# A routed two-layer mixture of experts: the second routing test of a phase written out among an expert's products, and the close of a phase split over two experts

## The reference, cut to what matters

```python
def _moe_ref(x, w_gate, w1, w2):          # N 3072, D 320, E 8, F 1024
    cap = N // E                          # 384
    flat = (x @ w_gate).flatten()
    for idx in np.argsort(-flat):         # greedy over all (token, expert) pairs
        tok, e = idx // E, idx % E
        if assigned[tok] >= 0 or counts[e] >= cap: continue
        assigned[tok] = e; counts[e] += 1
    for e in range(E):
        mask = assigned == e
        out[mask] = np.maximum(x[mask] @ w1[e], 0) @ w2[e]
```

## Time and profile before

| | |
|---|---|
| median of 3 runs | 870.5 us |
| lowest and highest | 869.16, 877.2 us |
| the profiled execution | 880.63 us |
| its span | 878.9 us |
| PE busy | 729.0 us (83%) |
| DVE, ACT, POOL busy | 529.1, 290.1, 413.2 us |
| mean granted TensorE clock | 0.90 of full speed |

### The profile page before, as it was taken

One profiled execution on the slowest core, in us unless ns is written; L12 is line 12 of the kernel. 1 busy time (PEld: TensorE's weight loads), 2 busy tenths in 40 slices (PEclk: granted clock), 3 DMA queues, 4 the chain that ended last, 5 costly groups with the idle time before them and its releaser, 6 DMA issues. The chain is left out here.

```text
span 878.9 us, 17001 instructions
## 1 busy us (share of the span) xinstructions
PE 729.0 (83%) x5044; PEld 672.5 (77%) x5044; DVE 529.1 (60%) x1622; ACT 290.1 (33%) x756; POOL 413.2 (47%) x557
## 2 busy tenths in 40 slices
PE   0999999994328795986959799983899998999897
PEld 0899999993217684866847698982899997999896
DVE  6479999985775556555556545445546364464462
ACT  4222222220014241422314246451524254245241
POOL 6568878871043452352426375874224043242341
PEclk9999999996558897897779799996899998999999
DMA  8857666625431411223221424535462424623610
GB/s 272 190 148 191 193 186 187 179 79 171 115 130 29 145 48 45 91 87 95 87 73 50 132 66 140 180 105 161 158 206 73 145 70 116 201 81 124 186 33 17
DMA packets 99641, 109.59 MB, mean 125 GB/s; under 512 B 39053, under 2 KB 83726, under 8 KB 99568
## 3 DMA queue, kind: packets, MB, share of 16 engines
q1 hardware_dynamic: 85792, 74.83, 29.8%
q10 hardware_dynamic: 9696, 21.24, 7.5%
q0 software_dynamic: 4080, 12.61, 4.5%
HBM read 89.45 MB, written 20.02 MB: 125 GB/s over the span
## 5 line engine op out<-in xcount | busy, mean ns | idle before, releaser
L535 POOL TENSOR_TENSOR parts_w2l<-all_w,parts_w2h 128x320 fp32r<-128x320 f32 x128 | 113.5, 903 | 131.2 <-ACT parts_w2h L522 128.2
L595 DVE SCALAR_TENSOR_TENSOR l_hl<-bank,l_hh 128x384 fp32r<-128x384 f32 (+1 forms) x168 | 83.1, 494 | 137.6 <-ACT l_hh L591 134.9
L591 ACT ACTIVATE l_hh<-bank 128x384 fp32r<-128x384 f32 (+1 forms) x168 | 74.0, 440 | 167.5 <-PE bank L576 163.0
L572 PE MATMUL bank<-l_xh,parts_w1h 128*128 128x384 f32 x256 | 94.8, 370 | 23.1 <-DVE l_xh L565 12.6
L573 PE MATMUL bank<-l_xl,parts_w1h 128*128 128x384 f32 x256 | 90.0, 352 | 0.0
L574 PE MATMUL bank<-l_xh,parts_w1l 128*128 128x384 f32 x256 | 89.8, 351 | 0.0
L529 POOL TENSOR_TENSOR parts_w1l<-all_w,parts_w1h 128x384 fp32r<-128x384 f32 x72 | 70.3, 1005 | 38.8 <-ACT parts_w1h L515 38.8
L1343 PE MATMUL bank<-parts_w2h,l_hh 128*128 128x320 f32 x192 | 74.4, 387 | 7.1 <-issue 7.1
L582 PE MATMUL bank<-parts_w2h,l_hh 128*128 128x320 f32 x232 | 74.5, 321 | 0.0
L572 PEld LDWEIGHTS bank<-l_xh,parts_w1h 128*128 128x128 f32 x256 | 50.9, 199 | 29.1 <-issue 15.2
L584 PE MATMUL bank<-parts_w2h,l_hl 128*128 128x320 f32 x232 | 71.6, 309 | 0.0
(11 more groups left out here) (253 smaller groups left out, 1900.5 us busy)
## 6 DMA issues: line engine op xcount, KB each, us to landing
all_w<-in_moe_w SPq DMA_DIRECT2D x10, 1280.0 KB, 6.3
all_w<-in_moe_w SPq DMA_DIRECT2D x10, 1024.0 KB
all_w<-in_moe_w ACTq DMA_DIRECT2D x6, 1280.0 KB, 12.5
att_kT<-in_kT SPq DMA_DIRECT2D x24, 256.0 KB, 2.8
att_qD<-in_qT SPq DMA_DIRECT2D x48, 128.0 KB, 3.1
att_qT<-in_qT SPq DMA_DIRECT2D x24, 256.0 KB, 3.1
all_w<-in_moe_w ACTq DMA_DIRECT2D x6, 1024.0 KB
all_w<-in_moe_w SPq DMA_DIRECT2D x20, 256.0 KB
```

What stands on the lines that cost most here:

```text
L535: ops.tensor_tensor(sh.w2l[:, r, p, :], sh.w2[:, p, :], sh.w2h[:, r, p, :].bitcast(FP), ALU.subtract).then_inc(sh.w2_low, 1)
L572: T.matmul(dst, sh.w1h[:, r, k, f], xh[:, k, :], start=k == 0, stop=False)
L591: return nc.scalar.activation(hh, src, ACT.Relu)
L595: return nc.vector.scalar_tensor_tensor(hl, src, 0.0, hh.bitcast(FP), ALU.max, ALU.subtract)
```

## The change

In each expert with a phase the test is now written twice in straight code, the first without the last two operations of `bounds` (`bounds(False)`); `any_inside`, `decide` and `more` follow the second, so the loop is entered only for a third round. `rnd` counts the tests, `asked` the decisions. `close(k)` stays at the end of expert e, behind all three row tiles, but `totals`, `listed_tokens` and `next_pivots` of that phase run in the up part of expert e + 1 (`before`). `listed_tokens(1)` moves likewise into expert 0. Eight other steps move with them: `places`, `ranks`, `route`, `gates`, `logits_tile`, `row_tile`, `list_bases` and `list_rows`. On POOL the scatter of e - 2 and then the gather of e + 1 stand between `low_w2(e)` and `low_w1(e + 1)`, and pieces 2 to 7 of `low_w1(0)` wait for the up products of expert 0.

```diff
@@ POOL
-            low_w1(0, range(FT))
+            low_w1(0, range(0, LATE))
+            for p in range(LATE, FT):
+                pool.wait_ge(up_psum, p - 1)
+                low_w1(0, (p,))
             for e in range(NE):
                 low_w2(e, range(0, 5))
-                if e + 1 < NE:
+                if e == NE - 2:
                     gather(e + 1)
                 low_w2(e, range(5, FT))
+                if e > 1:
+                    scatter(e - 2, range(CT), e - 2)
+                if e < NE - 2:
+                    gather(e + 1)
                 low_w1(e + 1, range(FT))
-                if e:
-                    scatter(e - 1, range(CT), e - 1)
+            scatter(NE - 2, range(CT), NE - 2)
@@ ACT
-                    if f == 2 and e + 1 < NE:
+                    if f == (2 if e == NE - 2 else 4 if e == NE - 3 else 5) and e + 1 < NE:
                         sides(e + 1)
...
+                    if e:
+                        exps(e - 1, slice(0, CT))
                     keep(e, 2)
@@ DVE, an expert
-                k = routes(e)
+                k, before = routes(e), e + 1 if e < NE - 2 else None
                 low_hidden(e, 0)
+                if before:
+                    listed_tokens(before)
                 low_hidden(e, 1)
-                if e + 1 < NE:
+                if before and before < NE - 2:
+                    next_pivots()
+                elif before:
+                    remaining(NE - 1)
+                if e == NE - 2:
                     list_bases(e + 1)
+                low_hidden(e, 2)
+                if e < NE - 2:
+                    list_bases(e + 1)
+                if e >= NE - 3:
+                    places(e - 2, e - 2, slice(0, CT), p_s[:, 32:32 + CT * NE])
                 if k:
                     matches()
-                low_hidden(e, 2)
+                low_hidden(e, 3)
                 if k:
                     choices()
-                low_hidden(e, 3)
+                low_hidden(e, 4)
+                if 1 < e < NE - 3:
+                    places(e - 2, e - 2, slice(0, CT), p_s[:, 32:32 + CT * NE])
                 if k:
                     compare(0)
...
                 if k:
                     reached()
-                    bounds()
+                if e < NE - 3:
+                    list_rows(e + 1)
+                if k:
+                    bounds(False)
+                    for i in range(AC):
+                        compare(i)
+                    reached()
                 if e + 1 < NE:
                     row_tile(e + 1, 0)
                 if k:
+                    bounds()
+                if e + 1 < NE:
+                    row_tile(e + 1, 1)
+                if e:
+                    route(e - 1, slice(0, CT), p_s[:, 0:CT * NE])
+                if k:
                     decide()
                     more()
...
                 if e + 1 < NE:
                     row_tile(e + 1, 2)
+                if k:
+                    close(k)
                 if e:
-                    places(e - 1, e - 1, slice(0, CT), p_s[:, 32:32 + CT * NE])
+                    gates(e - 1, e - 1, slice(0, CT))
@@ PE, an expert
                     if f == 1:
+                        if before:
+                            totals(before)
+                        if e > 1:
+                            ranks(e - 2)
+                    if f == (1 if e == NE - 2 else 3) and e + 1 < NE:
+                        list_bases(e + 1)
+                    if f == (5 if e < NE - 2 else 4) and NE - 3 <= e < NE - 1:
+                        list_rows(e + 1)
+                    if f == 3:
                         if k:
                             pe.wait_ge(pivots_ready, k + 1)
                             pivots()
...
+                        if (j, f) in ((0, 0), (0, 2), (0, 3), (0, 4)) and k:
+                            count(2 if f == 0 else f + 1)
+                        if (j, f) == (0, 2) and e < NE - 3:
+                            list_rows(e + 1)
+                        if (j, f) == (0, 5) and k:
                             codes()
+                        if (j, f) == (1, 0) and k:
+                            pivots_again()
+                        if (j, f) in (((0, 0), (0, 2), (0, 4)) if e == NE - 1 else ((1, 0), (1, 1), (1, 2))) and e:
+                            logits_tile(e - 1, f if j else f // 2)
+                        if (j, f) in ((1, 3), (1, 4), (1, 5), (1, 6), (1, 7), (2, 0)) and k:
+                            count(f - 3 if j == 1 else 5)
+                        if (j, f) == ((2, 1) if k else (1, 3)) and e + 1 < NE:
                             row_tile(e + 1, 0)
+                        if (j, f) == ((2, 4) if k else (1, 7)) and e + 1 < NE:
+                            row_tile(e + 1, 1)
+                        if (j, f) == (2, 2) and k:
+                            codes()
+                        if (j, f) == (2, 6) and k:
                             any_inside()
+                        if (j, f) == ((2, 7) if k else (2, 3)) and e + 1 < NE:
+                            row_tile(e + 1, 2)
+                        if (j, f) == (2, 7) and k:
                             decide()
                             more()
```

More of the change, by code:

```diff
@@ L864, in _ @@
             V.tensor_copy(pivot[:, :], best[:, 0:1])
-            go, rnd = dve.alloc_register("rt_go_v"), dve.alloc_register("rt_round_v")
+            go, rnd, asked = (dve.alloc_register(n) for n in ("rt_go_v", "rt_round_v", "rt_asked_v"))
             dve.reg_mov(rnd, 0)
+            dve.reg_mov(asked, 0)
             d()
@@ L917, in bounds @@
                 V.tensor_tensor(code[:, :], code[:, :], fresh[:, :], ALU.add)
+                dve.reg_add(rnd, rnd, 1)
+                if not closes:
+                    return
                 d()
@@ L923, in decide @@
             def decide():
-                dve.wait_ge(in_psum, dve.snap(rnd) + 1)
+                dve.wait_ge(in_psum, dve.snap(asked) + 1)
                 V.tensor_copy(flag[:, :], p_a[0:1, 0:1]).then_inc(flag_ready, 1)
@@ L928, in decide @@
                 dve.reg_load(go, flag[0:1, 0:1])
-                dve.reg_add(rnd, rnd, 1)
+                dve.reg_add(asked, asked, 1)
             def more():
@@ L1069, in low_hidden, with tail @@
                 hidden_low(nc, hl[:, f, :], hh[:, f, :], p_up[f % 2][:, 0:CAP]).then_inc(h_done, 1)
+            def tail(k):
+                listed_tokens(k)
+                if k < NE - 2:
+                    next_pivots()
+                else:
+                    remaining(NE - 1)
             for k in range(AHEAD):
@@ L1084, in _ @@
                 close(k)
-                listed_tokens(k)
-                next_pivots()
+                if k < AHEAD - 1:
+                    tail(k)
             for j in range(CT):
@@ L1128, in _ @@
                 if k:
+                    bounds()
[4 more added lines that the diff above has]
+                if k:
                     decide()
                     more()
[L1131 to L1134, removed]
-                    listed_tokens(k)
-                    if k < NE - 2:
-                        next_pivots()
-                    else:
-                        remaining(NE - 1)
                 if e + 1 < NE:
                     row_tile(e + 1, 2)
+                if k:
+                    close(k)
                 if e:
-                    places(e - 1, e - 1, slice(0, CT), p_s[:, 32:32 + CT * NE])
+                    gates(e - 1, e - 1, slice(0, CT))
+            places(NE - 2, NE - 2, slice(0, CT), p_s[:, 32:32 + CT * NE])
             for j in range(CT):
@@ L1167, in _ @@
             T = nc.tensor
-            go, rnd = pe.alloc_register("rt_go_p"), pe.alloc_register("rt_round_p")
+            go, rnd, asked = (pe.alloc_register(n) for n in ("rt_go_p", "rt_round_p", "rt_asked_p"))
             pe.reg_mov(rnd, 0)
+            pe.reg_mov(asked, 0)
             def pivots():
@@ L1185, in codes, with pivots_again @@
                 T.matmul(p_b[:, 0:P], code_w[:, :], reach[:, :], start=True, stop=True).then_inc(reach_psum, 1)
+                pe.reg_add(rnd, rnd, 1)
+            def pivots_again():
+                pe.wait_ge(inside_ready, pe.snap(rnd))
+                pe.sem_inc(pe_carry, 1)
+                pivots()
             def any_inside():
-                pe.wait_ge(inside_ready, pe.snap(rnd) + 1)
+                pe.wait_ge(inside_ready, pe.snap(rnd))
                 pe.sem_inc(pe_carry, 1)
@@ L1243, in _ @@
                 more()
-                totals(k)
+                if k < AHEAD - 1:
+                    totals(k)
             def result(e, j):
@@ L1308, in _ @@
             for e in range(NE):
-                r, k = e % 2, routes(e)
+                r, k, before = e % 2, routes(e), e + 1 if e < NE - 2 else None
                 for f in range(FT):
@@ L1324, in _ @@
                         result(e - 1, f // 2)
-                    if f == 4 and e + 1 < NE:
```

(9 more changed lines are left out.)

44 lines of the change are left out of this document (14 added, 30 removed).

## The result

The changed kernel takes **910.9 us** (median, 902.3 to 914.6) against 871.3 for the kernel before on the same chip: a ratio of 1.043, 95% interval 1.039 to 1.047. It is slower; my 880 had the sign, and a quarter of the size.

The account below looks back on a forecast made before the run. PE carries the chain of waits, with DVE's tests in the loop as the largest loss in the stage. Gains at the start and in experts 1 to 3 against losses elsewhere sum to +9.8 on 870.5: 880 us, range 858 to 893.

Parts of the forecast that it names:

- The start (-7.7): Before expert 0: thinned `low_w1(0)` frees the close's first operation, 5.7 us; moving the close's tail saves 2.0.
- The written order of an expert with two tests: Experts laid out operation by operation: 49.0 us for experts 2 to 4, 48.2 for expert 1, 44.5 for expert 0.
- The wait at the second pivots: Down part, first test: PE runs out of steps before DVE's inside result and idles 1.5 us.
- the loss beside GpSimd's pieces: Second bounds at an expert's end: DVE operations held by five low pieces, 0 to 3.2 us, taken at 2.6.
- the end chain: DVE's chain ending an expert, from row tile 0 to row tile 2: 9.9 to 10.3 us, 12.5 beside POOL's pieces.
- the price of the clock: Slower PE clock after the 1.5 us idle in the down part: 0 to 1.7 us, taken at 0.8.
- Expert 5 (+9.5): Expert 6's gather lands late, 3.6 us PE idle; slow start and longer DVE list; about +9.5 us with the clock.
- Expert 6 (+4.7): Late scatter of expert 4's rows delays `keep(6, 0)` and `row_tile(7, 0)`; `route(5)` meets POOL's pieces; +4.7 us, +1 to +6.
- Expert 7 (+2.0): One more scatter, 3.9 us, ahead of `low_w1(8)` and `low_w2(8)` on POOL; +2.0 us, 0 to 4.
- The rule against the term: Before expert 0: profile rows 5 show back-to-back pieces holding DVE, worth 5.7 us; the skill's one-piece lock would give 1.
- The fast one: Rival: end chain free of POOL and clock holds; experts 1 to 4 about 43.3 us, sum -23; chance 0.20, about 855.

Follow-up runs that it names:

- x4_thin: Kernel before with only pieces 2 to 7 of `low_w1(0)` waiting for expert 0's up products; 868.4 us, ratio 0.997 to the kernel before.
- x3_early: Changed kernel with all eight high pieces of w1 made by ScalarE ahead of `keep(e, 0)` in experts 0 to 4; 899.5 us.
- x2_fill: Changed kernel with the logits tiles of experts 1 to 4 moved to fill PE's wait for the second pivots; 884.9 us.
- y3_apart: Changed kernel with the second-pivots wait kept and the three logits tiles two steps later, behind the second test's first counts; 887.4 us.
- x6_pool: Changed kernel with GpSimd's order altered in experts 5 to 7: scatter behind the fifth low w2 half, expert 5's gather behind all eight; 897.6 us.
- x7_all: Changed kernel with three edits: logits in the second-pivots wait, high halves of w1 early, GpSimd's order in experts 5 to 7 altered; 863.1 us.
- z_last: x7_all with GpSimd's eight low halves of w2 for the second layer behind the three last scatters instead of ahead; 869.4 us.
- y2_before: Kernel before with thinned `low_w1(0)` and all eight high halves of w1 before the first result in experts with a test; 885.9 us.
- x5_both: Changed kernel with logits filling the second-pivots wait and all eight high halves of w1 made early in experts with a test; 872.5 us.

## Why the prediction was wrong

**The start (-7.7)**: right, -7.8, and for the reason given; x4_thin has the 5.7 of it alone, less 1.5 in expert 0.

**The written order of an expert with two tests**: right. The wait at the second pivots was 1.30 (forecast 1.5), the loss beside GpSimd's pieces 2.3 (2.6; x3_early confirms it), and expert 0, where no logits stand behind the wait, took 44.9 (44.5). x2_fill and y3_apart, in which the clock holds in the middle of the experts (but for 3.4 us in one), take 46.7 to 48.8 in experts 1 to 4, where I had 48.2 and 49.0. One sum in it is off by 0.2: the terms of the end chain give 9.7 to 10.1, not 9.9 to 10.3.

**The step that failed** is the price of the clock: "The 1.5 idle may bring a drop too: between 0 and 1.7, taken at 0.8." It cost 6.2, 7.1, 4.8 and 4.8 us in experts 1 to 4 (the same instructions against y3_apart), 22.9 in all where the sum had 3.2; that is 19.7 of the 21.0 that these experts are over my terms. The prediction gives no row for its bound of 1.7. Its one slow stretch is that of the earlier trace rows, 6.7 us behind a stop of 10.5, and it argues from the length of the stop ("no idle stretch is as long as the loop's 10.5"). The stop is short, but what follows it is three narrow logits tiles, and the stretch at 1.2 GHz is 10 to 17 us of products with PE full. Moving the logits takes 17 to 26 us off. The earlier trace rows is also only the part of its slow stretch in which PE has products: in the kernel before the clock is at its lower level from 340.7 to 354.4, which is 13.7 us. A bound from that length would have been half of it, 6.9 an expert, and so a rival with its own range.

**Expert 5 (+9.5)**: right, +10.5, with the wait for the gather at 4.07 (3.6).

**Expert 6 (+4.7)**: right in kind and too small, +7.2. I had the late scatter, not that the gather behind the fifth piece delays the last pieces of low w2 past the first down steps (1.39), nor the slow stretch that follows (expert 6 in the view by stretches):

```profile
571.20:584.80 13.60, 13.60 (x58) 13.37 (x57) 1.02 (x3) 2.99 (x8) 8.41 (x9) 0.53 0.42 134
```

**Expert 7 (+2.0)**: mis-sized, +6.4, and by another mechanism than the one I named. The scatter moved into this expert holds `keep(7, 0)` for 8.00 us, and `exps`, `gates` and the places stand behind it (PE waits 4.13 for the places, 2.26 in the kernel before). The pieces of w1 slide onto the routing (3.40 in place of 0.18). x6_pool moves the scatter back and expert 7 loses 4.0 of it.

**The rule against the term** went the way of rows 5: one operation of 0.17 us was held for 7.09 beside eight pieces in x7_all, 7.28 in z_last, 4.58 in y2_before, and 1.58 beside two. These operations waited out the whole run of pieces that was left. But not every run without a gap does that: the five pieces in expert 1 of the changed kernel fill 4.84 us without one, and each of the four operations beside them ended with a piece (0.40 to 1.08). There ScalarE had made each half at most 1.2 us before GpSimd took it, in y2_before 4.4 us before and more; that this is the difference isn't shown. The Trainium skill, SBUF — State Buffer, "SBUF: two separate sides", ties the lock to one instruction; the rows of 1.58 to 7.28 disagree with it there, and the four operations of expert 1 agree. The same section of the Trainium skill says that of VectorE's operations only those with two SBUF inputs or in a two-port mode take the pair; with the compares, which have one input in PSUM, the trace agrees (3.68 us beside the pieces in x7_all).

**The rivals.** The fast one ("the clock holds") was wrong in its condition; where the experiments meet its condition together with a free end (x5_both), experts 1 to 4 take 44.9 to 47.0, near its 43.3. Its own terms (2.6 and 3.1 in five experts, 2.3 in expert 5) add up to 30.8, so its sum is -21 and not -23. No rival was about a slow stretch in the middle of an expert.

## What to carry to other kernels

When TensorE gets a new short wait, look at what stands right behind it. Try wide products there, or fill the wait with the small matmuls (the two gave 21 and 26 us of 911 here), and judge by the granted clock of the stretch, not by idle time. When a list moves to a later place, follow each DMA that hangs on it to the first instruction that needs its data, and each queue position that it shifts: here the places of three scatters and one gather cost 8.6 us. A row of GpSimd pieces whose inputs are all ready should be laid beside operations that were seen not to be held by it (here compares on PSUM), and moving it elsewhere is no cure by itself.

## What the runs showed that I had not expected

- Six compares that read PSUM took 3.68 us beside back-to-back GpSimd pieces, as without; single operations on SBUF, of 0.15 to 0.18 us elsewhere, took 3.40 to 7.28.
- 10.2 to 17.0 us at 1.2 GHz with PE busy throughout, behind a stop of 1.30 us and logits; none behind the same stop with products first (y3_apart).
- An edit worth 12 us in one order of the instructions (x3_early) cost 15 us in the other (y2_before against x4_thin).
